# Operand sets made in the expert steps, and units that begin with three blocks per row group

## What is computed

```
q_p, k_p = phi(q), phi(k)                 # exp of +-(x @ w_phi - max)
num, den = q_p @ (k_p^T v), q_p @ sum(k_p)
x  = (num / den) as 2304 tokens x 512
e  = argmax(x @ w_gate)                   # one of 8 experts per token
y  = gate * relu(x @ w1[e]) @ w2[e]       # 512 -> 1024 -> 512
xn = y / rms(y) * rms_g
out = (silu(xn @ w_gate2) * (xn @ w_val)) @ w_out   # 512 -> 1536 -> 512
```

## Time and profile before

| | us |
|---|---|
| median of 3 runs | 937.08 (935.49 to 937.7) |
| profiled execution, time | 927.2 |
| its span | 925.6 |
| TensorE busy | 851.8 (92%) |
| VectorE busy | 530.2 (57%) |
| ScalarE busy | 359.0 (39%) |
| GpSimd busy | 197.6 (21%) |

### The profile page before, as it was taken

The page is one execution under the profiler, slowest core; times in us unless marked ns, Lnnn a source line. Parts: engine busy times, 40 slices in busy tenths (PEclk is TensorE's granted clock), DMA queues, the critical chain, the costliest instruction groups (busy, mean ns, idle before and its releaser), DMA issues.

```text
span 925.6 us, 16649 instructions
## 1 busy us (share of the span) xinstructions
PE 851.8 (92%) x6216; PEld 769.6 (83%) x6217; DVE 530.2 (57%) x931; ACT 359.0 (39%) x607; POOL 197.6 (21%) x211
## 2 busy tenths in 40 slices
PE   8999999999999999998672899999999678999997
PEld 6776868589999999998562799999999677888886
DVE  5688888998576333226664766666675484221220
ACT  4545555651454222224521543443443343222221
POOL 1011202034432122234604211111120120111011
PEclk9999999999999999999885999999999879999999
DMA  8615523023573212253007122222231623433430
GB/s 282 185 53 209 180 95 109 1 79 91 196 231 56 34 43 30 47 142 112 21 8 158 43 74 75 75 84 81 75 97 52 248 70 115 136 132 130 137 103 34
DMA packets 59755, 95.41 MB, mean 103 GB/s; under 512 B 8848, under 2 KB 42768, under 8 KB 57648
## 3 DMA queue, kind: packets, MB, share of 16 engines
q1 hardware_dynamic: 55392, 75.99, 28.5%
q0 software_dynamic: 3488, 17.85, 5.2%
q10 hardware_dynamic: 816, 0.79, 0.3%
HBM read 61.55 MB, written 33.08 MB: 102 GB/s over the span
## 4 chain that ended last, share of the span: by engine, by line
PE 76%; DVE 11%; issue 5%; DMA 3%; ACT 3%; POOL 1%; SPq 0%; POOLq 0%; ACTq 0%; DVEq 0%
PE ps L1138 8%; PE ps L1140 7%; PE ps L1139 7%; PE ps L1188 5%; PE ps L1190 5%; PE ps L1189 5%; PE ps L1049 4%; PE ps L1050 4%; PE ps L1051 4%; PE ps L1062 4%; PE ps L1064 4%; PE ps L1063 4%; PE ps L890 3%; PE ps L945 2%; PE ps L850 2%
## 5 line engine op out<-in xcount | busy, mean ns | idle before, releaser
L1138 PE MATMUL ps<-sH,upH 128*128 128x384 f32 x504 | 178.5, 354 | 53.9 <-ACT part L1424 28.7
L1139 PE MATMUL ps<-sL,upH 128*128 128x384 f32 x504 | 175.7, 349 | 0.0
L1140 PE MATMUL ps<-sH,upL 128*128 128x384 f32 x504 | 175.5, 348 | 0.0
L1138 PEld LDWEIGHTS ps<-sH,upH 128*128 128x128 f32 x504 | 99.7, 198 | 59.6 <-ACT part L1424 30.8
L1139 PEld LDWEIGHTS ps<-sL,upH 128*128 128x128 f32 x504 | 99.7, 198 | 0.1
L1140 PEld LDWEIGHTS ps<-sH,upL 128*128 128x128 f32 x504 | 99.4, 197 | 0.0
L1966 DVE TENSOR_TENSOR hTL<-h_st,hTH 128x768 fp32r<-128x768 f32 x36 | 32.9, 954 | 97.7 <-ACT hTH L1446 97.7
L1188 PE MATMUL ps<-woH,hTH 128*128 128x512 f32 x216 | 84.1, 389 | 2.4 <-DVE hTL L1966 2.4
L1742 DVE SCALAR_TENSOR_TENSOR hmL<-ps,hmH 128x288 fp32r<-128x288 f32 x64 | 29.2, 456 | 96.4 <-ACT hmH L1293 91.7
L1189 PE MATMUL ps<-woL,hTH 128*128 128x512 f32 x216 | 84.0, 389 | 0.0
L1190 PE MATMUL ps<-woH,hTL 128*128 128x512 f32 x216 | 84.0, 389 | 0.0
(11 more groups left out here) (238 smaller groups left out, 1782.5 us busy)
## 6 DMA issues: line engine op xcount, KB each, us to landing
h_dram<-hid SPq DMA_DIRECT2D x36, 384.0 KB, 2.7
h_st<-h_dram SPq DMA_DIRECT2D x18, 768.0 KB, 4.2
w_st<-in_ffn_up SPq DMA_DIRECT2D x14, 512.0 KB, 4.5
xin<-xs_dram SPq DMA_DIRECT2D x9, 578.2 KB, 8.2
xs_dram<-zrow SPq DMA_DIRECT2D x8, 578.2 KB, 7.6
qT<-in_q SPq DMA_DIRECT2D x4, 1152.0 KB, 6.1
xn_dram<-x2g SPq DMA_DIRECT2D x8, 576.0 KB, 5.5
xst<-xn_dram SPq DMA_DIRECT2D x3, 1536.0 KB, 8.6
```

What stands on the lines that cost most here:

```text
L1138: e.matmul(to, wh, xh, start=(fresh and c == 0), stop=False, skip_group_check=True)
L1139: e.matmul(to, wh, xl, start=False, stop=False, skip_group_check=True)
L1140: done = e.matmul(to, wl, xh, start=False, stop=(c == 1), skip_group_check=True)
```

## The change

Every expert step now also makes the whole operand set of one FFN block: SP loads 0.5 MB of its weights (`step_weights_in`), GpSimd makes the sums in three instructions (`weight_sums`), ScalarE the high parts in one (`weights_high`, at chunk 5), VectorE the low parts in one (`weights_low`, at chunk 6), and SP stores the set of 1.84 MB to a DRAM tensor (`weights_out`). The block's weights are stored on the host side in the order of the steps; slot `n` of the tensor holds block `n - 1`.

In the FFN stage blocks 0 to 5 are loaded from there, as operands (`operands_in`, two DMAs of four and three products), and so are the last three visits (blocks 0, 1, 2 again); three operand buffers take the place of two. Blocks 6 to 11 are still made in the FFN stage (`made_sums`, `made_high`, `made_low`, two parts each), two or three units or more ahead of their use and beside the units named in `MADE_AT`. The units begin with blocks 0, 1, 2 and group 0, the same with group 1, then blocks 3 to 8 with all groups, then 9 to 11 with each group, then 0 to 2 with group 2. The row operands are split beside the units named in `ROWS_AT`, the output weights one twelfth at a time beside units 30 to 34 (`OUT_AT`), and tile 0's rows beside unit 34. Group 2's load stands before the last token numbers' DMA. Buffers have moved: `homes`, `at_low`, `h_st`, `ysb`.

```diff
-UNITS = ([(q, sg) for sg in range(2) for q in range(2)] + [(q, sg) for q in range(2, NF - 2) for sg in range(NSG)]
-         + [(q, sg) for sg in range(NSG) for q in (NF - 2, NF - 1)] + [(NF, NSG - 1), (NF + 1, NSG - 1)])
+VISITS = (0, 1, 2, 3, 4, 5, 6, 7, 8, 9, 10, 11, 0, 1, 2)
+MADE = (6, 7, 8, 9, 10, 11)
+MADE_AT = {6: 10, 7: 13, 8: 16, 9: 19, 10: 22, 11: 25}
+UNITS = ([(v, sg) for sg in range(2) for v in range(3)] + [(v, sg) for v in range(3, 9) for sg in range(NSG)]
+         + [(v, sg) for sg in range(NSG) for v in (9, 10, 11)] + [(v, 2) for v in (12, 13, 14)])
+ROWS_AT = {(2, "A"): ((1, 0), (1, 1)), (2, "B"): ((1, 2),), (2, "C"): ((1, 3), (1, 4)), (3, "A"): ((1, 5),),
+           (3, "B"): ((1, 6),), (6, "A"): ((2, 0),), (6, "B"): ((2, 1),), (6, "C"): ((2, 2),), (7, "A"): ((2, 3),),
+           (7, "B"): ((2, 4),), (8, "A"): ((2, 5),), (8, "B"): ((2, 6),)}
+OUT_AT = {(30 + (n + 1) // 3, "ABC"[(n + 1) % 3]): n for n in range(NF)}
+TILE0_AT = {(34, "B"): 0, (34, "C"): 1}
...
             with e.Fori(0, total - 2) as n:
                 rows_next(n + 2)
+                step_weights_in(n + 1)
                 rows_out(n)
+                weights_out(n + 1)
             rows_next(total)
+            step_weights_in(last)
...
-            up_in(0)
+            e.wait_ge(s["e_st"], 16 * 8)
+            operands_in(0)
             e.wait_ge(s["xst"], total * 16)
             settle(e, "carry_sp")
             group_in(0)
             rows_out(prior)
+            e.wait_ge(s["e_lo"], total)
+            settle(e, "carry_sp")
+            operands_in(1)
+            e.wait_ge(s["pe_s1"], total * FC)
+            settle(e, "carry_sp")
+            operands_in(2)
...
             for u in range(2, NU):
                 hidden_out(u)
-                if u == last_of_group(0) + 2:
+                for vis in range(3, len(VISITS)):
+                    if vis not in MADE and last_of_visit(vis - 3) == u + 1:
+                        operands_in(vis)
+                    if vis == MADE[0] and u == 8 or vis in MADE[1:] and u == MADE_AT[MADE[nth_made(vis) - 1]]:
+                        weights_in(vis)
...
+                if u == last_of_group(0):
+                    e.wait_ge(s["pe_D"], u + 1)
                     for third in range(3):
                         e.dma_start(wo_st[:, third * 4:third * 4 + 4, :], ffn_out[:, third * 4:third * 4 + 4, :])\
                             .then_inc(s[f"wo_in{third}"], 16)
...
             def split_step(pair, par, g):
                 add_squares(g - 1)
                 gate_rows(g + 1)
                 with e.If(has_turn(pair * 2 + (par + 2))):
                     raw_in(1, pair * 2 + (par + 2), pair * (2 * PIECES) + ((par + 1) * PIECES + KC))
+                weight_sums(g)
+                with e.If(has_turn(pair * 2 + (par + 2))):
                     raw_in(2, pair * 2 + (par + 2), pair * (2 * PIECES) + (par + 2) * PIECES)
...
+            def weights_high(g):
+
+                e.wait_ge(s["e_add"], g * 3 + 3)
+                settle(e, "carry_act")
+                e.activation(tb[1][:, 0, :, :, :], t_raw[:, :, :, :], ACT.Copy).then_inc(s["e_hi"], 1)
...
+            def weights_low(g):
+
+                e.wait_ge(s["e_hi"], g + 1)
+                settle(e, "carry_dve")
+                e.tensor_tensor(tb[1][:, 1, :, :, :], t_raw[:, :, :, :], tb[1][:, 0, :, :, :].bitcast(F32), ALU.subtract)\
+                    .then_inc(s["e_lo"], 1)
...
             for u in range(2, NU):
                 first_copy(u)
                 first_sigmoid(u)
+                beside(u, "A")
                 second_sigmoid(u - 1)
                 second_copy(u)
+                beside(u, "B")
                 third_copy(u)
+                beside(u, "C")
```

More of the change, by code:

```diff
@@ L284, in build_program @@
             "normalised, stored; token numbers stored, read": "dve_xn xst idst id_in id_c",
+            "FFN up weights of a step: loaded, sums, operands split, stored": "e_in e_add e_hi e_lo e_st",
             "FFN rows loaded (one per group), their sums, operands split": "x_in0 x_in1 x_in2 s_add s_hi s_lo",
-            "FFN up weights loaded (one per staging buffer), their sums, operands split":
-                "w_in0 w_in1 w_in2 t_add t_hi t_lo",
+            "FFN up operands loaded (two parts per buffer)": "t_a0 t_a1 t_a2 t_b0 t_b1 t_b2",
+            "FFN up weights loaded, their sums, operands split (two parts each)": "w_in t_add t_hi t_lo",
             "a unit's products: the first, the second, sixth added, fifth added, fourth added": "pe_F pe_A pe_U pe_V pe_D",
@@ L1777, in _ @@
                 take_rows(0, XT_FIRST)
-                for name in ("dve_ms", "dve_R", "dve_xn"):
+                for name in ("dve_ms", "dve_R", "dve_xn", "e_lo"):
                     e.sem_inc(s[name], 1)
@@ new lines, in beside @@
+            def beside(u, pos):
+                before = slot_before(u, pos)
+                for sg, o in ROWS_AT.get(before, ()):
+                    row_low(sg, o)
+                for vis in MADE:
+                    if before[0] == MADE_AT[vis] and before[1] != "C":
+                        made_low(vis, "AB".index(before[1]))
+                if before in OUT_AT:
+                    out_low(OUT_AT[before])
+                if before in TILE0_AT:
+                    tile_rows_low(0, TILE0_AT[before])
@@ new lines, in _ @@
+            for o in range(4):
+                row_low(0, o)
+            first_gate(0)
+            for o in range(4, 7):
+                row_low(0, o)
+            values(0)
+            first_gate(1)
+            mean(total - 1, BANKS[1][3])
+            second_gate(0)
+            inverse(total - 1)
+            hidden_rows(0)
+            values(1)
+            normal(total - 1)
+            for u in range(2, NU):
+                first_gate(u)
+                beside(u, "A")
+                second_gate(u - 1)
+                beside(u, "B")
@@ L2034, in _ @@
-                if u == NU - 1:
-                    for half in range(2):
-                        tile_rows_low(0, half)
             second_gate(NU - 1)
```

428 lines of the change are left out of this document (189 added, 239 removed).

## The result

The changed kernel took 897.84 us (median; 896.75 to 899.18) where the kernel before took 936.29 in the same rounds: ratio 0.960, 95% interval 0.956 to 0.963. A second set of rounds gave 890.04 against 928.16, ratio 0.960 (0.957 to 0.964). It is faster by 4%, 38 us; forecast were 62.

A forecast was written before the change was run, and what follows sets the result against it. TensorE was taken to bound the kernel except in two stretches. Unit 35's values 59.9 us earlier plus 2.4 at the end gave 62.3; 937.1 - 62.3 = 874.8, rounded 875, range 866 to 889.

The forecast's parts named there:

- The experts, "3 us": Seven expert steps: added work costs 1.2 us in each of two split steps, 0.15 in five plain ones, 3 in all.
- VectorE is late already, so all 2.0 go on, less some 0.8: Two weight-splitting expert steps: VectorE's new 2.0 us subtraction lacks idle time before it, so each step loses 1.2 us.
- ring: An expert step's store, load, sums and two splits of FFN weights: closed at 21 of the step's 27.2 us.
- rival (B): Expert steps: the ring outlasts the step, deciding from a 16 us store on; slower than before, 937 to 950; chance 0.03.
- The store, "8 to 10 us": Expert steps: 1.84 MB store takes 8 to 10 us, load 4.5, so weights are there 9 to 10 into next step.
- Unit 0: First FFN unit: starts at 432.0, waits 0.3 us for the first copy and some 1 for low parts, ends 439.6.
- Units 1 to 3, "1.6 and 0.8 us": Early FFN units: TensorE loses 1.6 us in unit 2 to ScalarE's high parts, 0.8 in unit 3 to VectorE.
- (A): Before unit 3: waits return as DMA waits, group 1's rows land at 460, unit 3 10 us later; 887; chance 0.22.
- Unit 10, "3.5 and 2 of half clock": First block made in FFN stage: late load stalls TensorE 3.5 us, half clock adds 2, 5.5 in all.
- SP's new waits end 4 us into a unit, so nothing queues behind them.: FFN units: SP's waits for a free operand buffer end before the unit's hidden rows are to be stored; no cost.
- (C): Expert steps and made blocks: splits hold TensorE for all 14 us, five more 3.5 us stalls; 903; chance 0.05.
- (D): Unit 10: no stall, as the load lands in its least, 4.0 us, and units keep pace; 868; chance 0.10.

The follow-up runs named there:

- the second profile: The changed kernel run again with nothing edited, against the kernel before: 890.04 against 928.16 us, ratio 0.960, span 885.8.
- the best version: Changed kernel plus third hidden-row buffer and first made block's load behind unit 7: 874.32 us against 931.90 for the kernel before, ratio 0.9375.

## Why the prediction was wrong, step by step

The direction was right and the size was not: the range of 866 to 889 doesn't hold 897.8. The steps that failed most are in the units: a small store's wait was put at nothing, and VectorE's instructions were priced from a row with GpSimd idle. By the second profile, which has the undisturbed start, the error of 22.5 us in the span is 3.8 in the expert steps, 3.0 in unit 0, 8.8 in units 0 to 4 and 7.3 behind them. The 9.9 us added for the profile's distance from the median is no property of the kernel: the two sets of rounds gave medians of 936.3 and 928.2 for the kernel before.

**The attention stage and the end.** Taken as unchanged: right (scatter of 7 us apart). The end gains 2.7 us (2.4 forecast).

**The experts, "3 us".** They cost 6.8: the last product of the experts starts at 438.0, where I had the end at 431.2 without the change. The plain steps cost nothing (27.2 us), as argued. The two split steps were priced at 1.2 each and cost 2.8 and 1.8. "VectorE is late already, so all 2.0 go on, less some 0.8" was nearly right: 1.6 us are seen in the first step when the instruction is left out, and none in the second. The failed step is what I put at nothing, the store as a neighbour: 1.3 us in the first step and 1.2 at the turn's boundary are issue gaps that go when the store moves. The second step's ring closes late because the raw weights of an expert are loaded beside it: the rows landed there 16.3 us after their issue, against 10.1 to 11.9 in the steps behind. This is like rival (B) in one step of seven, but not by the store's time as I had put it: it was to decide from a store of 16 us on, and there the trace has 10.9 us and, with the order changed, 17.9. Of the rest 0.65 us lie in the last step, where VectorE's low part took 2.94 us beside GpSimd's sums for the FFN rows; without these sums it took 2.02 and TensorE had no gap. Steps of 27.2 to 28.5 us were the sign of being right; three of the six listed were longer.

**The store, "8 to 10 us", weights there "9 to 10 us into the next step".** The store was too short, without effect in the plain steps: 10.3 to 12.4 us from its issue, 23.1 us into a step, to that of the load behind it, and 3.2 to 3.6 to land, so the weights are there 8.2 to 11.5 us into the next step. (The prediction's own terms give 7.3 to 9.3.) What they wait for, GpSimd's gating, ends at 10.2 to 12.0.

**Unit 0.** Two waits, 0.3 and some 1 us, were forecast. There were three, 1.9, 0.95 and 0.9: ScalarE starts its high parts at 438.3, where the products of unit 0 could start, and not before the experts' end; then the low parts beside GpSimd's squares took twice their time (two in 4.12 us). In the first profile half clock came on top, 4 us.

**Units 1 to 3, "1.6 and 0.8 us".** The largest failed step. I had taken 0.95 us for VectorE's instructions from the earlier trace rows, a row with GpSimd idle, although GpSimd's sums for group 1's rows, 8.9 us, had to fall into this very stretch; the prediction has them only under (A). Without the sums 5.2 of the 8.8 us go (3.4 to 5.9 by the other pairs). Most of the rest is unit 3 to 4 (11.3 us also without the sums), where the sigmoid waits 6.4 us for the store of unit 2's hidden rows; unit 4 is the first with a third buffer, and there it takes 9.4 us.

**Unit 10, "3.5 and 2 of half clock".** The stall was 3.2 to 3.5 us in every profile with the late load: right in place, cause and size. The half clock came behind it in seven of eleven such profiles and not in the other four, the first profile among these (below); where it came in the second, units 10 to 11 took 1.5 us longer (8.35 against 6.89).

**"SP's new waits end 4 us into a unit, so nothing queues behind them."** True of the queue, and it looked only at the queue. A store of hidden rows that is issued while operand, row or output-weight loads ahead of it are still in flight takes 6 to 8 us, and the price of this was put at nothing. The prediction has no row of the store: 2.7 us as a median in the kernel before hides one of 11.0 us, and 2.8 to 2.9 in the changed kernel the three of 6.3 to 8.3. The chain in the first profile, ScalarE then TensorE, two units behind such a store:

```profile
498.89 0.52 ACT L1491 ACTIVATE hid<-gate 128x384 f32<-128x384 f32 x1 [6.63 <-DMA h_dram<-hid]
...
500.26 0.69 PE L1224 MATMUL ps<-sH,tb 128*128 128x384 f32 x1 [3.23 <-ACT part L1507]
...
715.57 0.52 ACT L1491 ACTIVATE hid<-gate 128x384 f32<-128x384 f32 x1 [6.82 <-DMA h_dram<-hid]
...
717.46 0.44 PE L1224 MATMUL ps<-sH,tb 128*128 128x384 f32 x1 [3.99 <-ACT part L1507]
```

The third buffer is worth 10 to 12 us from unit 4 on, more than the 7.3 missing there. By luck the pace was priced too high: 31 units at 7.39 are 229.1 us, and the best version takes 226.0. About 1 of these 3 us is the wait for the store inside the pace (0.04 per unit); where the rest lies is open.

**Rivals.** (A) had the right resource, the 16 DMA engines, but the wrong victim: group 1's rows did take 15.9 us to land (8.6 was the median in the earlier trace rows), at 455.4, and their sums began there, yet TensorE waited at most 0.7 us for a part made of them; the larger loss came from a small store. That transfers of all issuers interleave on the same engines, which I cited for (A) from the Trainium skill, "DMA: Bandwidth & Descriptors", Issuing engines are not separate DMA queues, fits the second step, where SP's rows took 16.3 us beside raw weights that GpSimd's queue loads. (C) named the splits: VectorE's share of 1.6 us is a ninth of its 14, and no profile has a gap at the other five made blocks. (D), no stall at unit 10, didn't occur, and its condition could not have brought it about: a load 0.5 us shorter takes 0.5 us off a stall of 3.5.

## What to carry to other kernels

When a change adds large transfers to a stretch, ask of every small transfer there who waits for it two steps on, not only who stands behind it in its queue; a buffer more for that one was worth 10 to 12 us here, more than any new order of the queue gave. What counts is what is in flight ahead of it when it is issued. Take the duration of a VectorE instruction from a row with GpSimd in the state that it will have. And a pace taken over many units is an upper bound of the bottleneck's own pace, until the waits of the other engines inside it are gone. Before a difference between two profiles is put down to an edit, look at how far the same stretch scatters in profiles that don't have the edit.

## Not expected of the hardware

**The clock after the same stall.** TensorE restarts unit 0 after 1.86 us of idle time in both profiles of the changed kernel, and waits again within 6 us. First profile, then the stretches 454 to 458 there and 442 to 446 in the second (us; busy of PE, PEld, DVE, ACT, POOL; PEclk; DMA share; GB/s):

```profile
451.14 0.44 PE L1224 MATMUL ps<-sH,tb 128*128 128x384 f32 x1 [1.86 <-DVE sL L1990]
...
453.66 0.69 PE L1224 MATMUL ps<-sH,tb 128*128 128x384 f32 x1 [1.15 <-DVE sL L1990]
...
454.00:458.00 4.00, 3.48 (x11) 2.97 (x11) 4.00 (x2) 1.16 (x2) 3.64 (x3) 0.50 1.02 408
```

```profile
442.00:446.00 4.00, 3.05 (x17) 2.73 (x17) 3.79 (x4) 3.41 (x6) 3.30 (x2) 1.00 1.01 408
```

At 0.50 (1.2 GHz) unit 0's values came 13.2 us after its first product, at 1.00 (2.4 GHz) 9.4; over the fifteen profiles of the changed kernel and its edits it was 9.4 in five, and 11.8 to 13.4 in ten. In unit 10 the same stall was followed by full clock in the first profile (1.00 from 548 to 562 us) and by half clock from 0.5 us behind the restart in the second:

```profile
549.52 0.44 PE L1224 MATMUL ps<-sH,tb 128*128 128x384 f32 x1 [3.35 <-ACT part L1507]
```

```profile
537.37 0.44 PE L1224 MATMUL ps<-sH,tb 128*128 128x384 f32 x1 [3.33 <-ACT part L1507]
...
538.00:540.00 2.00, 2.00 (x8) 2.00 (x7) 1.76 (x3) 0.54 (x2) 0.00 (x0) 0.50 0.04 8
```

So the rule that I had read from two restarts in the earlier trace rows, half clock after 2.6 us and not after 1.5, is none: the length of a stall doesn't decide alone, and some 4 us of scatter come from it. The trace of the kernel before had shown it already. Two more of its restarts:

```profile
435.03 0.44 PE L1138 MATMUL ps<-sH,upH 128*128 128x384 f32 x1 [3.51 <-DVE sL L1928]
...
524.38 0.44 PE L1138 MATMUL ps<-sH,upH 128*128 128x384 f32 x1 [2.63 <-ACT part L1424]
```

Both first matmuls ran at full clock, and half clock came all the same: some 1.3 us behind the first restart, and within 1 us of the second (a mean of 0.74 from 524 to 526 us, 0.50 from 526 to 528). So the first matmul doesn't tell what follows either. On this point the Trainium skill, "TensorE: Matmul & The Clock Gate", Part 1 on the clock gate, whose advice to leave the ramp out I had set aside, adds that the count of slow matmuls at a kernel's start varies from run to run; these rows show the like in the middle of one.

**Time for which nothing is waited.** A store of 1.84 MB in flight went with a longer issue gap at a boundary of the program: 3.7 instead of 2.1 us on ScalarE and 1.7 instead of 0.5 on TensorE; with the store moved behind the boundary both were short again. No transfer of the instruction queues stands near it, and the cause is open.
